# Routing rounds over ten packed slots instead of 24 tiles, in a fused attention and mixture-of-experts kernel

## Chip, cores and metric

The kernel runs on one core of one Trainium2 chip. The metric is the device time of one execution in microseconds, the median of several runs. All times of the kernel before are of that kernel on such a core.

## The reference

The program computes three layers, the second of which has a routing that depends on the data.

```python
# 1: attention with a decaying state, batch 4, 8 heads, 768 steps, head_dim 48
state = alpha[:, :, t, :, None] * state + outer(k[:, :, t], v[:, :, t])
y[:, :, t] = q[:, :, t] @ state
# 2: x = y as (3072 tokens, 384); E = 8 experts, F = 1024
logits = x @ w_gate                 # (3072, 8)
order = np.argsort(-logits.flatten())
for idx in order:                   # greedy, best pair first
    tok, e = idx // E, idx % E
    if assigned[tok] >= 0 or counts[e] >= cap: continue      # cap = 384
    assigned[tok] = e; counts[e] += 1
out[assigned == e] = relu(x[assigned == e] @ w1[e]) @ w2[e]
# 3: on every token, d_ff = 1536
g = x @ w_gate2
return (silu(g) * (x @ w_val)) @ w_out
```

So every expert ends up with exactly 384 tokens, and which ones depends on the order of 24,576 numbers.

## The kernel before

**Stages.** `attention` computes layer 1 and the logits, which stay on the chip as `logits`, 128 partitions by 24 tiles (`TILES`) by 8 experts; token 128·t + p lies on partition p in tile t. `layers` then takes the experts one after the other, in the order in which the routing fills them: layer 2 and layer 3 for the 384 tokens of that expert, and the rows go to `out`.

**Greedy routing as phases.** Since the best pairs go first, the routing is eight phases. In a phase every free token has one choice, its best expert among those with room (`choose`, L863 to L878: `best`, and `choice` as one of eight marked). The phase looks for the threshold on `best` at which the first expert becomes full, and assigns every token at or over it (`take`, L848). Phase 0, in front of the experts, uses four rounds of 31 cuts (`first_rounds_vector`). Phases 1 to 7 use three rounds (`FINE_ROUNDS`) of 99 cuts. A round has four parts: DVE compares `best` of each tile with all cuts (`compare`, L736, into `at_row`), PE counts per cut and expert with one small matmul for each of the 24 tiles (L891, into `ps_count`), DVE sees which cuts fill an expert (`find_full`, L744), PE sums these over partitions (L896), and DVE moves the base of the search (`raise_base`, L751). After `take`, the tokens of the newly full expert are ranked and listed: DVE writes a 128-wide row of marks per tile (L829, two halves of 12 tiles) and 24 matmuls (L911, two stretches of 12) turn them into token numbers, `slot_token`. On DVE nearly every small operation goes through `link`, which waits for the one before it.

**Where a phase runs.** The phase p+1 is spread over the work of expert p as steps s, in code written out by hand (`vector_step`, `tensor_step`, called by `route`). An expert has 20 places for a step. Places 0 to 7 come in the loop over m, the eight slices of layer 2: PE does `up(m+1)`, `down(m)` (9 matmuls each), then the step m; DVE makes `h_low(m)`, then the step m. Places 8 to 19 come in the loop over j, the twelve slices of layer 3: PE does `gate_and_value(j+1)` (18 matmuls), `project(j)` (9), then the step 8+j; DVE makes two products and `u_low(j)`, then the step. The phase takes 16 steps: compare, compare and count, find, three times; at s = `TAKE` = 9 `take`; then room and order (10), ranks (11), a first part of `at_row` (12) and a second (13), `slot_token` (14) and `choose` (15); the remaining small parts of phase p+1 lie in the same steps. `down(m)` waits for `h_low(m)` and `project(j)` for `u_low(j)`, so a step that keeps DVE too long makes PE wait.

**Other engines.** ACT makes the high parts of the numbers (each float32 matmul is three matmuls of split numbers), SP loads the weights. POOL subtracts to make `w_low` (L1438), starts the indirect transfers that gather the tokens of the next expert (L1430) and store those of the last (L1461), and in the first expert makes all of `gated_low` (L1296). `order[p]` tells SP which weights to load, at s = TAKE+1; `slot_token` releases the gather.

**A second way.** If at the end the routing did not come out exactly (`check_vector`: room left or below zero, a phase that filled no expert or two, a token left free), a second, exact routing and all the experts run again.

## Time and profile before

| | before |
|---|---|
| median of 3 runs | 874.03 us (872.48 to 876.46) |
| the profiled execution | 874.86 us |
| its span, first to last instruction | 873.0 us |
| PE busy | 835.8 us (96%) |
| DVE / ACT / POOL busy | 558.7 / 280.0 / 276.8 us |
| an expert, from the second on | 86.0 to 86.4 us |
| DMA, mean | 88 GB/s |

Attention fills the first 135 us or so, the first phase of the routing lies between it and about 168 us, and the eight experts fill the rest. To read it: the page's totals say which engine is busy, the stretches cut along the experts say whether that engine has any gap there, and the order of instructions in time says what a gap waits for. Spans of PE instructions overlap, so costs on PE are taken from the distance between starts.

### The profile page before, as it was taken

What the parts mean: (1) busy time and instruction counts of PE and PEld (TensorE: products, weight loads), DVE (VectorE), ACT (ScalarE), POOL (GpSimd) and SP (SyncE); (2) the same over time, 40 slices, a digit from 0 to 9 for tenths busy, and PEclk for the clock granted to TensorE, in tenths of its full rate; (3) what the DMA queues carried; (4) which work ended last, traced back from release to release, by engine and by line L of the source; (5) the groups of instructions that cost most, each with busy time, mean ns of one, the idle gap of its engine ahead of it and who ended that gap; (6) DMA issues with size and microseconds to landing.
All of it is one profiled execution on the core that took longest, in us unless ns stands there. A gap on an engine that the chain in (4) does not pass through costs nothing.

```text
span 873.0 us, 17172 instructions
## 1 busy us (share of the span) xinstructions
PE 835.8 (96%) x6425; PEld 792.0 (91%) x6425; DVE 558.7 (64%) x1065; ACT 280.0 (32%) x505; POOL 276.8 (32%) x263
## 2 busy tenths in 40 slices
PE   8899995699989999999999999999999999999995
PEld 5788884499989999999999999999999999999995
DVE  8999986757865665566556755675567556742332
ACT  1344443322323333333333333333333323333221
POOL 3222210179736041604150515051506050604001
PEclk9999997799999999999999999999999999999998
DMA  8899952500320041004100410031013001300000
GB/s 328 292 355 357 319 201 90 172 1 1 110 63 27 0 126 45 27 0 134 37 27 6 134 36 22 20 126 34 18 37 116 27 18 48 105 28 19 1 1 30
DMA packets 26001, 77.25 MB, mean 88 GB/s; under 512 B 3824, under 2 KB 10480, under 8 KB 23152
## 3 DMA queue, kind: packets, MB, share of 16 engines
q1 hardware_dynamic: 19440, 62.67, 20.8%
q0 software_dynamic: 3072, 9.44, 3.2%
q10 hardware_dynamic: 3456, 4.72, 1.5%
q8 instruction: 18, 0.29, 0.1%
q14 instruction: 15, 0.12, 0.0%
HBM read 67.38 MB, written 9.44 MB: 88 GB/s over the span
## 4 chain that ended last, share of the span: by engine, by line
PE 74%; DVE 6%; issue 2%; ACT 1%; DMA 0%; POOL 0%; POOLq 0%; DVEq 0%; ACTq 0%
PE ps_up L1634 44%; PE ps_acc L1634 27%; PE ps_turn_again L891 1%; DVE quick_at_row L829 1%; DVE u_low L1602 1%; DVE act_out L1599 1%; ACT u_high L1538 1%; PE ps_turn L1640 1%; PE ps_turn_again L911 0%; DVE act_out L1595 0%; PE ps_turn_again L771 0%; DVE quick_at_row L741 0%; DMA x_tok<-x_rows,slot_token 0%; PE ps_up L1640 0%; POOL x_tok L1493 0%
## 5 line engine op out<-in xcount | busy, mean ns | idle before, releaser
L1438 POOL TENSOR_TENSOR w_low<-w_raw,w_high 128x384 fp32r<-128x384 f32 x120 | 150.4, 1280 | 229.8 <-ACT w_high L1519 228.8
L1634 PE MATMUL ps_up<-z_high,gated_high 128*128 128x384 f32 x576 | 199.2, 346 | 0.2 <-DVE z_low L1590 0.2
L1634 PE MATMUL ps_up<-z_high,gated_low 128*128 128x384 f32 x576 | 195.5, 339 | 0.0
L1634 PE MATMUL ps_up<-z_low,gated_high 128*128 128x384 f32 x576 | 193.0, 335 | 0.0
L1538 ACT CAST u_high<-act_out 128x384 fp32r<-128x384 f32 x96 | 49.2, 513 | 190.9 <-DVE act_out L1599 190.9
L1634 PEld LDWEIGHTS ps_up<-z_high,gated_high 128*128 128x128 f32 x576 | 108.4, 188 | 0.6 <-issue 0.5
L1634 PEld LDWEIGHTS ps_up<-z_high,gated_low 128*128 128x128 f32 x576 | 108.5, 188 | 0.0
L1634 PEld LDWEIGHTS ps_up<-z_low,gated_high 128*128 128x128 f32 x576 | 108.3, 188 | 0.0
L1634 PE MATMUL ps_acc<-gated_high,u_high 128*128 128x384 f32 x288 | 97.6, 339 | 3.0 <-DVE u_low L1602 3.0
L1634 PE MATMUL ps_acc<-gated_high,u_low 128*128 128x384 f32 x288 | 97.1, 337 | 0.0
L1634 PE MATMUL ps_acc<-gated_low,u_high 128*128 128x384 f32 x288 | 97.0, 337 | 0.0
L1595 DVE TENSOR_TENSOR act_out<-ps_up,act_out 128x384 f32<-128x384 f32 x96 | 53.5, 557 | 67.5 <-ACT act_out L1535 63.8
L1461 POOL DMA_INDIRECT out<-o_tok,to_rows x24 | 26.0, 1085 | 220.6 <-ACT o_tok L1547 186.0
L1602 DVE TENSOR_TENSOR u_low<-act_out,u_high 128x384 fp32r<-128x384 f32 x96 | 58.3, 608 | 55.6 <-ACT u_high L1538 55.6
L1535 ACT ACTIVATE act_out<-ps_up 128x384 f32<-128x384 f32 x96 | 47.0, 490 | 129.9 <-PE ps_up L1634 129.9
L1584 DVE SCALAR_TENSOR_TENSOR h_low<-ps_up,h_high 128x384 fp32r<-128x384 f32 x64 | 35.6, 556 | 70.4 <-ACT h_high L1515 70.3
L1599 DVE TENSOR_TENSOR act_out<-act_out,ps_up 128x384 f32<-128x384 f32 x96 | 53.3, 555 | 38.6 <-PE ps_up L1634 37.2
L1634 PE MATMUL ps_up<-x_high,w_high 128*128 128x384 f32 x192 | 67.9, 354 | 1.1 <-ACT x_high L1511 1.1
L1519 ACT CAST w_high<-w_raw 128x768 fp32r<-128x768 f32 x64 | 53.3, 834 | 47.5 <-PE ps_acc L1634 35.0
L741 DVE SCALAR_TENSOR_TENSOR quick_at_row<-quick_best,quick_base,quick_fine_cuts 128x1485 bf16<-128x1485 f32 (+1 forms) x42 | 65.7, 1565 | 0.5
L1634 PE MATMUL ps_up<-x_high,w_low 128*128 128x384 f32 x192 | 65.2, 340 | 0.0
L1634 PE MATMUL ps_up<-x_low,w_high 128*128 128x384 f32 x192 | 65.1, 339 | 0.0
(179 smaller groups left out, 1467.6 us busy)
## 6 DMA issues: line engine op xcount, KB each, us to landing
w_raw<-in_experts SPq DMA_DIRECT2D x64, 384.0 KB, 3.0
qka_in<-in_qka SPq DMA_DIRECT2D x22, 1026.0 KB, 7.8
gated_raw<-in_gated SPq DMA_DIRECT2D x12, 576.0 KB, 6.8
v_in<-in_v SPq DMA_DIRECT2D x24, 192.0 KB, 7.0
x_rows<-y_rows ACTq DMA_DIRECT2D x24, 192.0 KB, 5.4
qka_in<-in_qka SPq DMA_DIRECT2D x2, 512.0 KB, 6.4
qka_in<-in_qka SPq DMA_DIRECT2D x1, 514.0 KB, 6.5
out<-o_tok,to_rows POOLq DMA_INDIRECT x24, 2.6
```

Of the source, the lines that this page charges most:

```text
L741: dve.scalar_tensor_tensor(out=self.at_row[:, tiles, 0:n], in0=self.best[:, tiles].unsqueeze(2).broadcast_to(tc), scalar=self.base[:, 0:1] ...
L829: dve.tensor_tensor(self.at_row[:, tiles, :], self.row[:, tiles].unsqueeze(2).broadcast_to(half), self.row_numbers[:, :].unsqueeze(1).broa ...
L1438: part = pool.tensor_tensor(w.low[:, m % RING, cols], w.raw[:, m % RING, cols], w.high[:, m % RING, cols].bitcast(F32), ALU.subtract)
L1461: pool.indirect_dma_start(out=out, out_offset=bass.IndirectOffsetOnAxis(ap=to_rows[:, t:t + 1], axis=0), in_=o_tok[:, t, :], in_offset=Non ...
L1519: act.copy(w.high[:, m % RING, :], w.raw[:, m % RING, :]).then_inc(w_high_ready, 1)
L1535: act.activation(act_out[:, j % 2, :], ps_up[j % 2][0][:, 0:CAP], ACT.Sigmoid).then_inc(sigm_ready, 1)
L1538: act.copy(u_high[:, j % 2, :], act_out[:, j % 2, :]).then_inc(u_high_ready, 1)
L1584: dve.scalar_tensor_tensor(out=h_low[:, m % 2, :], in0=ps_up[m % 2][0][:, 0:CAP], scalar=0.0, in1=h_high[:, m % 2, :].bitcast(F32), op0=AL ...
L1595: dve.tensor_tensor(act_out[:, j % 2, :], ps_up[j % 2][0][:, 0:CAP], act_out[:, j % 2, :], ALU.mult).then_inc(silu_ready, 1)
L1599: dve.tensor_tensor(act_out[:, j % 2, :], act_out[:, j % 2, :], ps_up[j % 2][1][:, 0:CAP], ALU.mult).then_inc(gated_ready, 1)
L1602: dve.tensor_tensor(u_low[:, j % 2, :], act_out[:, j % 2, :], u_high[:, j % 2, :].bitcast(F32), ALU.subtract).then_inc(u_low_ready, 1)
L1634: mm = pe.matmul(acc, lhs[a], rhs[b], start=(first and i == 0), stop=(last and i == 2))
```

## The change

From phase 1 on, the rounds no longer go over 24 tiles. Two new steps at the front of the phase (`SEARCH = 2`) pack the free tokens of each partition into ten slots. Step 0: `free` marks tokens whose `best` is a real number, a running sum gives each its place 1, 2, ..., `held` marks for slot j the tile whose free token has place j, and `number` is the choice as a number 1 to 8. Step 1: two products with `held` and two sums give `slot_best` and `slot_number`, and one comparison gives `slot_choice`. The compare then covers ten slots in one instruction and the count is ten matmuls. Compare and count lie in one step now, so a round has two steps instead of three. `TAKE` is 8 instead of 9, and each later step runs one place earlier. The matmuls of the listing, 12 in step TAKE+3 and 12 in TAKE+4 before, all run in TAKE+4. A partition with more than ten free tokens would have the rest left out of the counts.

```diff
-FINE_TILES = (slice(0, 15), slice(15, TILES))
+SLOTS = 10
...
-    TAKE = 3 * FINE_ROUNDS
+    SEARCH = 2
+    TAKE = SEARCH + 2 * FINE_ROUNDS
...
 # vector_step
-        n = s // 3
-        if s % 3 == 0 and 0 < s <= take:
+        n, finding = divmod(s - self.SEARCH, 2)
+        by_slot = [P, SLOTS, TILES]
+        if s == 0:
+
+            link(dve.tensor_scalar(self.free, self.best[:], -0.1 * BIG, None, ALU.is_gt))
+            link(dve.tensor_tensor_scan(self.place, self.free, self.zeros[:], 0.0, ALU.add, ALU.add))
+            link(dve.tensor_tensor(self.place, self.place, self.free, ALU.mult))
+            link(dve.tensor_tensor(self.held, self.place.unsqueeze(1).broadcast_to(by_slot),
+                                   self.numbers[:, 1:SLOTS + 1].unsqueeze(2).broadcast_to(by_slot), ALU.is_equal))
+            link(dve.tensor_tensor(self.numbered, self.choice[:],
+                                   self.numbers[:, 1:E + 1].unsqueeze(1).broadcast_to(te), ALU.mult))
+            link(dve.tensor_reduce(self.number, self.numbered, AX_X, ALU.add))
+        if s == 1:
+            for of, into in ((self.best[:, :], self.slot_best), (self.number, self.slot_number)):
+                link(dve.tensor_tensor(self.held_part, self.held, of.unsqueeze(1).broadcast_to(by_slot), ALU.mult))
+                link(dve.tensor_reduce(into[:], self.held_part, AX_X, ALU.add))
+            se = [P, SLOTS, E]
+            link(dve.tensor_tensor(self.slot_choice[:], self.slot_number[:, :].unsqueeze(2).broadcast_to(se),
+                                   self.numbers[:, 1:E + 1].unsqueeze(1).broadcast_to(se), ALU.is_equal))
+        if self.SEARCH < s <= take and not finding:
             self.raise_base(dve, self.rounds_before(p) + n, self.fine_cuts[:, n - 1, 0:1])
-        if s % 3 < 2 and s < take:
-            self.compare(dve, FINE_TILES[s % 3], self.fine_cuts[:, n, :])
-        if s % 3 == 2 and s < take:
+        if self.SEARCH <= s < take and not finding:
+            self.compare(dve, self.slot_best[:, :], slice(0, SLOTS), self.fine_cuts[:, n, :])
+        if self.SEARCH <= s < take and finding:
             self.find_full(dve, self.rounds_before(p) + n + 1, FINE_CUTS - 1)
...
 # tensor_step
-        if s % 3 == 1 and s < take:
-            for i, tiles in enumerate(FINE_TILES):
-                pe.wait_ge(self.over_cut_ready, 2 * self.rounds_before(p) + 2 * n + i + 1)
-                for t in range(tiles.start, tiles.stop):
-                    mm = pe.matmul(self.ps_count, self.at_row[:, t, :], self.choice[:, t, :],
-                                   start=(t == 0), stop=(t == TILES - 1))
+        if self.SEARCH <= s < take and not finding:
+
+            pe.wait_ge(self.over_cut_ready, ROUNDS + self.rounds_before(p) + n + 1)
+            for j in range(SLOTS):
+                mm = pe.matmul(self.ps_count, self.at_row[:, j, :], self.slot_choice[:, j, :],
+                               start=(j == 0), stop=(j == SLOTS - 1))
...
-        if s in (take + 3, take + 4):
-            i = s - take - 3
-            pe.wait_ge(self.at_row_ready, 2 * p + i + 1)
+        if s == take + 4:
+            for i in range(2):
+                pe.wait_ge(self.at_row_ready, 2 * p + i + 1)
```

Three places in the order of instructions show it; the numbers of lines shift by up to 30 in the kernel after. On PE, in the loop over m, the first count stands behind `down(1)` before:

```order
L1634 MATMUL ps_acc<-h_low,w_high 128x384
L889 ISA
L891 MATMUL ps_turn_again<-quick_choice,quick_at_row 128x8 x15
L889 REGISTER_ALU
L891 MATMUL ps_turn_again<-quick_choice,quick_at_row 128x8 x9
L1700 REGISTER_ALU
L1634 MATMUL ps_up<-x_high,w_high 128x384
```

and behind `down(2)` in the kernel after:

```order
L1664 MATMUL ps_acc<-h_low,w_high 128x384
L919 ISA
L921 MATMUL ps_turn_again<-quick_slot_choice,quick_at_row 128x8 x10
L1730 REGISTER_ALU
L1664 MATMUL ps_up<-x_high,w_high 128x384
```

Two waits and 24 matmuls became one wait and ten. On DVE, at the start of an expert, before:

```order
L1584 SCALAR_TENSOR_TENSOR h_low<-ps_up,h_high 128x384
L741 SCALAR_TENSOR_TENSOR quick_at_row<-quick_best,quick_base,quick_fine_cuts 128x15x99
L1583 REGISTER_ALU
L1584 SCALAR_TENSOR_TENSOR h_low<-ps_up,h_high 128x384
L741 SCALAR_TENSOR_TENSOR quick_at_row<-quick_best,quick_base,quick_fine_cuts 128x9x99
```

and after (the register and ISA rows are the waits of `link`; the scratch tiles lie in unused columns of `at_row` and bear its name):

```order
L1614 SCALAR_TENSOR_TENSOR h_low<-ps_up,h_high 128x384
L799 TENSOR_SCALAR quick_at_row<-quick_best 128x24
L694 ISA
L800 SCALAR_TENSOR_TENSOR quick_at_row<-quick_at_row,quick_zeros 128x24
L694 REGISTER_ALU
L801 TENSOR_TENSOR quick_at_row<-quick_at_row 128x24
L694 REGISTER_ALU
L802 TENSOR_TENSOR quick_at_row<-quick_at_row,quick_numbers 128x240
L694 REGISTER_ALU
L804 TENSOR_TENSOR quick_at_row<-quick_choice,quick_numbers 128x192
L694 REGISTER_ALU
L806 TENSOR_REDUCE quick_at_row<-quick_at_row 128x24
```

A compare of 15 tiles in the first place has become six small operations, and five more stand in the second. On DVE, behind the first `u_low` of layer 3 (j = 0), before:

```order
L1595 TENSOR_TENSOR act_out<-ps_up,act_out 128x384
L1599 TENSOR_TENSOR act_out<-act_out,ps_up 128x384
L1602 TENSOR_TENSOR u_low<-act_out,u_high 128x384
L747 REGISTER_ALU
L748 TENSOR_TENSOR quick_fills<-ps_turn_again,quick_room_or_big 99x8
```

and after:

```order
L1625 TENSOR_TENSOR act_out<-ps_up,act_out 128x384
L1629 TENSOR_TENSOR act_out<-act_out,ps_up 128x384
L1632 TENSOR_TENSOR u_low<-act_out,u_high 128x384
L765 SCALAR_TENSOR_TENSOR quick_base<-ps_turn_again,quick_fine_cuts,quick_base 128x1
L694 REGISTER_ALU
L882 TENSOR_SCALAR quick_is_over<-quick_best,quick_base 128x24
L694 REGISTER_ALU
L883 TENSOR_TENSOR quick_got<-quick_choice,quick_is_over 128x192
```

The find of the last round was there; now the last `raise_base` and `take` are, which stood behind `u_low` of j = 1 before.

## Rows read from the trace of the kernel before

**Rows 1.** page, busy time of the engines (share of the span).
```profile
PE 835.8 (96%) x6425; PEld 792.0 (91%) x6425; DVE 558.7 (64%) x1065; ACT 280.0 (32%) x505; POOL 276.8 (32%) x263
```

**Rows 2.** first, second expert: us; PE, PEld, DVE, ACT, POOL busy; clock; DMA.
```profile
172.00:262.39 90.39, 86.21 (x572) 83.23 (x571) 61.84 (x103) 26.88 (x49) 63.30 (x57) 1.00 0.15 48
262.39:348.80 86.41, 86.41 (x581) 84.76 (x580) 53.08 (x104) 28.46 (x50) 27.02 (x24) 1.00 0.16 50
```

**Rows 3.** timeline of PE, waits in the first expert (start, us, what [idle, releaser]).
```profile
217.47 0.19 PE L904 MATMUL ps_turn_again<-quick_mine,quick_below 128*128 128x24 bf16 x1 [1.24 <-DVE quick_mine L800]
...
221.37 0.41 PE L1634 MATMUL ps_acc<-gated_high,u_high 128*128 128x384 f32 x1 [0.42 <-DVE u_low L1602]
...
248.58 0.41 PE L1634 MATMUL ps_acc<-gated_high,u_high 128*128 128x384 f32 x1 [2.28 <-DVE u_low L1602]
```

**Rows 4.** timeline of PE, second expert, around its first count.
```profile
270.09 0.76 PE L891 MATMUL ps_turn_again<-quick_choice,quick_at_row 128*128 128x8 bf16 x24
...
270.97 0.34 PE L1634 MATMUL ps_up<-x_high,w_low 128*128 128x384 f32 x1
271.14 0.34 PE L1634 MATMUL ps_up<-x_low,w_high 128*128 128x384 f32 x1
```

**Rows 5.** timeline of PE, second expert, first half of its listing.
```profile
316.93 0.46 PE L911 MATMUL ps_turn_again<-quick_token_parts,quick_at_row 128*128 128x6 bf16 x12
...
317.50 0.34 PE L1634 MATMUL ps_up<-z_high,gated_low 128*128 128x384 f32 x1
```

**Rows 6.** timeline of DVE, start of the second expert.
```profile
264.54 0.56 DVE L1584 SCALAR_TENSOR_TENSOR h_low<-ps_up,h_high 128x384 fp32r<-128x384 f32 x1 [1.48 <-ACT h_high L1515]
265.01 1.76 DVE L741 SCALAR_TENSOR_TENSOR quick_at_row<-quick_best,quick_base,quick_fine_cuts 128x1485 bf16<-128x1485 f32 x1
...
267.15 1.14 DVE L741 SCALAR_TENSOR_TENSOR quick_at_row<-quick_best,quick_base,quick_fine_cuts 128x891 bf16<-128x891 f32 x1
```

**Rows 7.** DVE groups of the second expert (busy us, mean ns | idle).
```profile
L876 DVE TENSOR_TENSOR quick_fine_cuts<-quick_numbers,quick_fine_step 128x297 f32<-128x297 f32 x1 | 0.5, 471 | 0.0
...
L869 DVE TENSOR_REDUCE quick_best<-quick_limited 128x24 f32<-128x192 f32 x1 | 0.4, 353 | 0.0
...
L811 DVE TENSOR_TENSOR quick_rank<-quick_rank,quick_mine 128x24 f32<-128x24 f32 x1 | 0.2, 184 | 0.0
```

**Rows 8.** timeline of PE, second expert, beginnings: down(1), up(4), project(1).
```profile
268.52 0.33 PE L1634 MATMUL ps_acc<-h_high,w_high 128*128 128x384 f32 x1
...
273.99 0.42 PE L1634 MATMUL ps_up<-x_high,w_high 128*128 128x384 f32 x1
...
300.90 0.34 PE L1634 MATMUL ps_acc<-gated_high,u_high 128*128 128x384 f32 x1
```

**Rows 9.** timeline of POOL, second expert.
```profile
270.98 1.99 POOL L1438 TENSOR_TENSOR w_low<-w_raw,w_high 128x384 fp32r<-128x384 f32 x2
...
317.47 3.30 POOL L1438 TENSOR_TENSOR w_low<-w_raw,w_high 128x384 fp32r<-128x384 f32 x2 [1.43 <-ACT w_high L1519]
```

**Rows 10.** timeline of DVE, first expert, around take.
```profile
202.97 0.56 DVE L1602 TENSOR_TENSOR u_low<-act_out,u_high 128x384 fp32r<-128x384 f32 x1 [0.58 <-ACT u_high L1538]
...
203.94 0.56 DVE L1595 TENSOR_TENSOR act_out<-ps_up,act_out 128x384 f32<-128x384 f32 x1
...
206.13 0.64 DVE L1602 TENSOR_TENSOR u_low<-act_out,u_high 128x384 fp32r<-128x384 f32 x1 [0.58 <-ACT u_high L1538]
...
207.72 1.12 DVE L853 TENSOR_TENSOR quick_got<-quick_choice,quick_is_over 128x192 bf16<-128x192 bf16 x1
...
210.91 0.56 DVE L1595 TENSOR_TENSOR act_out<-ps_up,act_out 128x384 f32<-128x384 f32 x1
```

**Rows 11.** timeline of DVE, second expert, the same operations.
```profile
298.38 0.36 DVE L853 TENSOR_TENSOR quick_got<-quick_choice,quick_is_over 128x192 bf16<-128x192 bf16 x1
298.77 0.50 DVE L856 TENSOR_REDUCE quick_got_rows<-quick_got 128x8 bf16<-128x192 bf16 x1
...
299.58 0.26 DVE L861 TENSOR_TENSOR quick_assigned<-quick_assigned,quick_got 128x192 bf16<-128x192 bf16 x1
```

More of the change, by code:

```diff
@@ L510 @@
 STEPS = (1 << BITS) - 1
-QUICK_LINKS = 38
+QUICK_LINKS = 49
 EXACT_LINKS = 8 + 4 + 6 * (DIGITS - 1) + 17
@@ L584, in __init__ @@
         self.at_row = sb("at_row", [P, TILES, P], BF16)
+        self.slot_best = sb("slot_best", [P, SLOTS])
+        self.slot_number = sb("slot_number", [P, SLOTS])
+        self.slot_choice = sb("slot_choice", [P, SLOTS, E], BF16)
+        words = self.at_row[:, SLOTS:TILES, :].rearrange("p a b -> p (a b)").bitcast(F32)
+        self.held = words[:, 0:SLOTS * TILES].rearrange("p (j t) -> p j t", j=SLOTS)
+        self.held_part = words[:, SLOTS * TILES:2 * SLOTS * TILES].rearrange("p (j t) -> p j t", j=SLOTS)
+        rest = words[:, 2 * SLOTS * TILES:]
+        self.numbered = rest[:, 0:TILES * E].rearrange("p (t e) -> p t e", t=TILES)
+        self.free, self.place, self.number = (rest[:, TILES * (E + n):TILES * (E + n + 1)] for n in range(3))
         self.lows = sb("lows", [P, B, CH - 1])
@@ L735, in rounds_before, with compare @@
         return FINE_ROUNDS * p + ROUNDS - FINE_ROUNDS
-    def compare(self, dve, tiles, cuts):
+    def compare(self, dve, best, tiles, cuts):
         n = cuts.shape[-1]
         tc = [P, tiles.stop - tiles.start, n]
-        dve.scalar_tensor_tensor(out=self.at_row[:, tiles, 0:n], in0=self.best[:, tiles].unsqueeze(2).broadcast_to(tc),
+        dve.scalar_tensor_tensor(out=self.at_row[:, tiles, 0:n], in0=best.unsqueeze(2).broadcast_to(tc),
                                  scalar=self.base[:, 0:1], in1=cuts.unsqueeze(1).broadcast_to(tc),
@@ L761, in first_rounds_vector @@
             for i in range(2):
-                self.compare(dve, slice(i * TILES // 2, (i + 1) * TILES // 2), self.cuts[:, n, :])
+                tiles = slice(i * TILES // 2, (i + 1) * TILES // 2)
+                self.compare(dve, self.best[:, tiles], tiles, self.cuts[:, n, :])
             self.find_full(dve, n + 1, CUTS - 1)
@@ L832, in vector_step @@
         if s == take + 5:
[L833 removed]
+            dve.wait_ge(self.tokens_ready, p + 1)
             with self.nc.allow_low_precision(reason="token numbers up to N are exact"):
```

13 lines of the change are left out of this document (6 added, 7 removed).

## The prediction, made blind

> **What bounds the kernel now.** I read the page first: TensorE is busy for 96% of the span and VectorE for 64% [rows 1]. A share over the whole span mixes stages, so I cut it along the experts. From its first `up` to its last `project` the second expert takes 86.41 us, and PE is busy for all 86.41 of them, at a granted clock of 1.00, the upper of its two levels, 2.4 GHz [rows 2]. The five experts after it look the same. There is no gap on PE to close in there: a change pays by what it takes out of PE's stream, and costs what it adds in waits. The first expert is different: PE is busy 86.21 of 90.39 us [rows 2], and the timeline of PE says why. It waits 1.24 us for the `mine` of the routing, then 0.42 and 2.28 us for `u_low` [rows 3]. There VectorE is late, and it is the only expert in which POOL is busy for most of the time (63.30 us against 27.02 [rows 2]). So there are two questions: how many nanoseconds of PE one small matmul is worth, and whether VectorE's new work stays inside its cover.
>
> **What leaves PE.** A count of 24 matmuls starts at 270.09 and the second matmul behind it starts at 270.97. Ordinary starts lie 0.17 apart (270.97 to 271.14), so the count costs 0.88 - 0.17 = 0.71 us [rows 4]. Half a listing, 12 matmuls of the same kind, costs 317.50 - 316.93 - 0.17 = 0.40 us [rows 5]. The difference, 0.31 us for 12, is 0.026 us for each matmul, and 0.09 us is left as the price of switching over and back. Ten matmuls should then cost 0.35 us, and a count gives back 0.36 us. There are 3 rounds in each of 7 phases: 21 x 0.36 = **7.6 us**. The listing as one stretch costs 0.71 in place of 0.80 us: 7 x 0.09 = **0.6 us**. The second matmul of each round (L896) only moves. Phase 0 keeps its rounds; its listing waits for the same two halves as before, so nothing changes there. Together 8.2 us, all on the path, as PE has no other gap.
>
> **What VectorE gets, from the second expert on.** The packing has eleven operations. None has a row of its own, so I bound them by the nearest: 0.18 us for 24 elements, 0.35 us for a sum over 192, 0.47 us for 297 [rows 7]; 240 elements lie between, about 0.41. With 0.03 us between linked operations (298.38 + 0.36 to 298.77 [rows 11]) step 0 takes 3 x 0.2 + 0.41 + 2 x 0.36 + 0.2 = 1.9 us, between 1.7 and 2.2, and step 1 takes 4 x 0.41 + 0.25 + 0.15 = 2.0 us. `h_low(0)` ends at 265.10 [rows 6], so step 0 ends at 267.0, `h_low(1)` at 267.6, and `down(1)` starts at 268.52 [rows 8]: cover 0.9 us. Step 1 then ends at 269.6 and `h_low(2)` at 270.2, while `down(2)` comes two times nine matmuls after `down(1)`, at 271.6: cover 1.4 us. The compare of ten slots has 990 elements, between 1.14 us for 891 and 1.76 us for 1485, nearest the lower: 1.25 us [rows 6], and it replaces both. Priced at nothing.
>
> In layer 3 each step stands one place earlier, so `take` comes behind `u_low(0)` instead of `u_low(1)`. In the second expert `take` and the `raise_base` ahead of it run from 297.9 to 299.84 [rows 11], 2.0 us. In the new place the next product waits 1.6 us for it, `u_low(1)` ends at about 299.5, and `project(1)` starts at 300.90 [rows 8]: cover 1.4 us, nothing on PE. `order` and `slot_token` are ready one step earlier. That makes nobody faster, because SP's loads and POOL's gather are paced by free weight buffers and by POOL's own `w_low`.
>
> **What it does to the first expert.** There `take` lasts from 206.77 (206.13 + 0.64) to 210.91, 4.1 us [rows 10]. In its old place the product after it would have been due one slice of PE later than the one at 203.94, that is 27 x 0.175 = 4.7 us, at about 208.7; it came 2.2 us late. In the new place `take` starts when `u_low(0)` ends, 203.53, the product is due at 203.94 [rows 10], and it comes some 3.7 us late. VectorE thus reaches the heavy steps of room and ranks 1.5 us further behind, while PE reaches them 1.1 us earlier (three counts). I carried that chain on with the times of the rows: waits of 0.3, 1.3, 1.9 and 0.6 us in place of 1.24 and 0.42, some 2.4 us more. Against this, the last routing step now stands one place earlier, and the wait of 2.28 us behind it [rows 3] shrinks or goes. The ends are 2.4 us lost and 2.3 us won; I take half of the late wait as gone: **1.2 us lost**.
>
> **Sum.** 8.2 - 1.2 = 7.0 us. Against the profiled execution, 874.86 us (span 873.0), that is 867.9; that execution is 0.8 us over the median of the runs, 874.03, so the median should be 867.0.
>
> **Contention, a rule against the row.** First the rows: the same product of 192 elements takes 0.36 us in the second expert [rows 11] and 1.12 us in the first [rows 10], where POOL subtracts without a pause, while nothing else about it differs. The Trainium skill, "SBUF — State Buffer", section "Who interferes with whom", states that a VectorE instruction with two inputs in SBUF and a GpSimd instruction that reads SBUF exclude each other for a whole instruction, and that `tensor_reduce` is free of it. By that rule most operations of the packing can be held, and the trace agrees with the rule in the 0.76 us between the two rows. Whether it bites depends on what POOL does during steps 0 and 1. The first `w_low` of the second expert starts at 270.98 [rows 9], after both steps (269.6). In the first expert POOL is subtracting by step 1, at most one instruction of 1.0 us in the way, within the cover of 1.4 us.
>
> **Rivals.**
> 1. *The packing and the compare push POOL or VectorE out of cover in the later experts.* `w_low` for `up(4)` is done at 270.98 + 1.99 = 272.97, and `up(4)` starts at 273.99 [rows 8, 9]; after the change it starts 0.36 us earlier, at 273.6. The compare of step 2 now lies at 270.2 to 271.5, so `w_low` may begin only at 271.5 and end at 273.5: 0.1 us of cover. If VectorE gets between its two halves, they take 3.30 us, as the pair at 317.47 did [rows 9], and end at 274.3. PE then waits 0.7 us in six experts, 4.2 us: 867.0 + 4.2 = 871.2. For it speaks the thin cover, against it that the compare is likely under way before POOL begins. Chance 0.20.
> 2. *The first expert wins.* If VectorE catches up before its last routing step, PE keeps its savings and the 2.28 us [rows 3] go as well: 874.0 - 8.2 - 2.3 = 863.5. The cheaper compare (1.25 for 2.90 us in each round) speaks for it, the chain above against it. Chance 0.18.
> 3. *Slower: the packing is held in every expert.* If the stores that POOL starts in steps 0 and 1 hold VectorE as its subtraction does, four or five operations of step 0 each take 0.76 us more, up to 3.8 us, of which 0.9 us is covered. PE waits 2.9 us in each of seven experts, 20 us: about 887. It decides from 1.8 us of waits per expert on, where the 8.2 us and the 4.4 us of a visible loss are used up. Against it: what POOL has in those steps are starts of stores, and its first subtraction comes at 270.98 [rows 9]. Chance 0.05.
> 4. *It doesn't do what it says.* If a partition had over ten free tokens, a phase would take too many, the check at the end would find it, and all the experts would run again: over 1500 us. I followed the reference's own assignment on its inputs of seed 0: 248 tokens are free after phase 0, at most 5 of them in one partition. Chance 0.01.
>
> **How the numbers follow.** The case of the sum has a chance of 0.56 and its own range from 865 to 869. The range from 863.0 to 871.5 takes in rivals 1 and 2, and leaves out rivals 3 and 4 and their edges. A measurement of this kernel can tell about 0.5% from no change, 4.4 us, so "faster" ends at 869.7. Faster: 0.53 of the first case, all of rival 2, a quarter of rival 1: 0.76. Slower: rivals 3 and 4: 0.06. Within 0.5%: 0.18.
>
> **What would show it.** The group of counts should have 210 matmuls for 504, and a count should cost about 0.35 us between starts. An expert should last 85.3 us for 86.4, with PE busy throughout. The first expert should show larger waits of PE for `mine` and for `u_low` around 205 to 220 us, and a smaller one before 250. The packing's groups should sum to 3.9 us per expert. A wait of `down(1)` for `h_low` or of `up(4)` for `w_low` in every expert would make the prediction wrong, and so would a price per matmul that falls well under 0.026 us at ten in a row.

## The result, and the profile after

The kernel after takes **907.13 us** (median of 3 runs, 906.96 to 907.15), against 874.03 before: a ratio of **1.0375** (95% interval 1.0344 to 1.0406). It is slower, and far outside the predicted range of 863.0 to 871.5 us.

The page of the kernel after: span, busy time, two of the rows of 40 slices, and the chain that ended last.

```profile
span 905.3 us, 16689 instructions
...
PE 840.9 (93%) x6131; PEld 795.5 (88%) x6131; DVE 577.3 (64%) x1121; ACT 280.3 (31%) x505; POOL 251.8 (28%) x263
...
PE   8899993897998999899989998999899989999996
...
PEclk9999996899998999899989998999899989999998
...
PE ps_up L1664 41%; PE ps_acc L1664 23%; DVE quick_at_row L752 5%; DMA out<-o_tok,to_rows 1%; PE ps_turn_again L921 1%; DVE quick_at_row L809 1%; PE ps_turn_again L941 1%; DVE z_low L1620 1%; PE ps_turn L1670 0%; ACT z_high L1562 0%; DVE quick_at_row L859 0%; PE ps_turn_again L783 0%; ACT h_high L1545 0%; DMA x_tok<-x_rows,slot_token 0%; DVE act_out L1629 0%
```

PE executes 294 instructions fewer than before [rows 1], as announced, and yet its busy share fell from 96% to 93%. From the thirteenth slice on (about 272 us, the second expert), one slice in every four has a lower PE digit and a lower clock digit. Four slices are about one expert, so something happens once per expert. A compare, L752, now holds 5% of the chain. The waits of PE in the kernel after (us in total, times, the longest) name the place:

```profile
PE ps_turn_again L921 <- DVE quick_at_row L752: 25.7, 6, 4.3
...
PE ps_acc L1664 <- DVE u_low L1632: 3.5, 4, 1.5
PE ps_turn_again L934 <- DVE quick_mine L830: 3.3, 2, 1.8
```

The first line has no counterpart before. In each of the experts two to seven the first count, the one of step 2, waits 4.28 us for its compare. Here is DVE in the second expert (start, us, what):

```profile
268.82 0.24 DVE L812 TENSOR_TENSOR quick_slot_choice<-quick_slot_number,quick_numbers 128x80 bf16<-128x80 f32 x1
269.19 0.56 DVE L1614 SCALAR_TENSOR_TENSOR h_low<-ps_up,h_high 128x384 fp32r<-128x384 f32 x1
269.66 7.53 DVE L752 SCALAR_TENSOR_TENSOR quick_at_row<-quick_slot_best,quick_base,quick_fine_cuts 128x990 bf16<-128x990 f32 x1
277.12 0.55 DVE L1614 SCALAR_TENSOR_TENSOR h_low<-ps_up,h_high 128x384 fp32r<-128x384 f32 x1
...
283.18 1.25 DVE L752 SCALAR_TENSOR_TENSOR quick_at_row<-quick_slot_best,quick_base,quick_fine_cuts 128x990 bf16<-128x990 f32 x1
```

The same instruction takes 1.25 us in the next round and 7.53 us here. Below, a VectorE operation is called *held* where it takes longer than its usual time while POOL works. POOL at that time:

```profile
269.37 0.96 POOL L1491 DMA_INDIRECT out<-o_tok,to_rows  x1 [2.43 <-DMA out<-o_tok,to_rows]
270.35 5.79 POOL L1468 TENSOR_TENSOR w_low<-w_raw,w_high 128x384 fp32r<-128x384 f32 x6
283.81 1.50 POOL L1468 TENSOR_TENSOR w_low<-w_raw,w_high 128x384 fp32r<-128x384 f32 x1 [7.67 <-ACT w_high L1549]
```

The compare starts while POOL starts its last store. POOL then subtracts six times without a gap, up to 276.14, and the compare ends 1.05 us after that, at 277.19. PE at that time (at 277.25, the count; behind it, big matmuls):

```profile
272.63 0.34 PE L1664 MATMUL ps_acc<-h_low,w_high 128*128 128x384 f32 x1
277.25 0.43 PE L921 MATMUL ps_turn_again<-quick_slot_choice,quick_at_row 128*128 128x8 bf16 x10 [4.28 <-DVE quick_at_row L752]
...
278.00 0.52 PE L1664 MATMUL ps_up<-x_high,w_low 128*128 128x384 f32 x1
278.32 0.52 PE L1664 MATMUL ps_up<-x_low,w_high 128*128 128x384 f32 x1
```

The windows of the same stretch (from, to, length; PE, PEld, DVE, ACT, POOL busy; granted clock, share of DMA, GB/s):

```profile
273.00:277.20 4.20, 0.00 (x0) 0.00 (x0) 4.20 (x2) 0.83 (x1) 3.14 (x4) 0.73 0.00 0
277.20:280.00 2.80, 2.75 (x18) 2.75 (x19) 0.79 (x3) 0.00 (x0) 0.00 (x0) 0.50 0.00 0
280.00:282.00 2.00, 2.00 (x9) 2.00 (x7) 0.56 (x1) 0.49 (x1) 0.00 (x0) 0.56 0.00 0
282.00:284.00 2.00, 2.00 (x13) 1.84 (x13) 1.04 (x2) 0.84 (x1) 0.19 (x1) 1.00 0.00 0
```

The wait has a second price. PE is idle for 4.28 us, its granted clock falls to 0.50, the lower level (1.2 GHz), and matmuls start 0.32 us apart instead of 0.17 until shortly before 282. From there on the clock is back at 1.00, 2.4 GHz. The later experts repeat this: from the first `up` of one expert to the first `up` of the next, the experts two to seven take 91.49 to 92.17 us, against 86.39 to 86.41 before. Summed over the six, that is 33.2 us. The first expert got 0.22 us shorter (93.32 to 93.10). So the six account for the whole loss (32.3 us between the spans).

**Why POOL's run has no gap now.** POOL in the second expert of the kernel before, around the second compare:

```profile
270.98 3.92 POOL L1438 TENSOR_TENSOR w_low<-w_raw,w_high 128x384 fp32r<-128x384 f32 x4
275.06 4.09 POOL L1438 TENSOR_TENSOR w_low<-w_raw,w_high 128x384 fp32r<-128x384 f32 x2 [0.17 <-ACT w_high L1519]
```

DVE of the same kernel there:

```profile
274.44 2.04 DVE L741 SCALAR_TENSOR_TENSOR quick_at_row<-quick_best,quick_base,quick_fine_cuts 128x1485 bf16<-128x1485 f32 x1
```

POOL has to wait for ACT's third `w_high` behind four subtractions, 0.17 us, and the compare of 15 tiles that arrived at 274.44 is done at 276.48. ACT makes the `w_high` that goes with `w_low` for a weight buffer after PE has left that buffer, behind a `down`. In the kernel after, `down(2)` stands ahead of the first count, so ACT has the third `w_high` ready in time (each is enough for two subtractions) and POOL has six subtractions to do instead of four. The fourth `w_high` needs `down(3)`, which stands behind the count, which needs the compare, which needs POOL to pause: a ring that opens only when POOL has run out of ready work.

### The profile page after: what moved, and what is told of

Same layout as the page of the kernel before. It is cut to its first block, busy times and chain, and to the rows that moved or that the text cites. A ratio compares the mean times of both kernels' runs of the same rounds, so it can differ in the third digit from the quotient of the medians.

```text
span 905.3 us, 16689 instructions
## 1 busy us (share of the span) xinstructions
PE 840.9 (93%) x6131; PEld 795.5 (88%) x6131; DVE 577.3 (64%) x1121; ACT 280.3 (31%) x505; POOL 251.8 (28%) x263
## 4 chain that ended last, share of the span: by engine, by line
PE 66%; DVE 12%; issue 3%; ACT 1%; DMA 1%; POOL 1%; POOLq 0%; DVEq 0%; ACTq 0%
PE ps_up L1664 41%; PE ps_acc L1664 23%; DVE quick_at_row L752 5%; DMA out<-o_tok,to_rows 1%; PE ps_turn_again L921 1%; DVE quick_at_row L809 1%; PE ps_turn_again L941 1%; DVE z_low L1620 1%; PE ps_turn L1670 0%; ACT z_high L1562 0%; DVE quick_at_row L859 0%; PE ps_turn_again L783 0%; ACT h_high L1545 0%; DMA x_tok<-x_rows,slot_token 0%; DVE act_out L1629 0%
## 5 line engine op out<-in xcount | busy, mean ns | idle before, releaser
L1468 POOL TENSOR_TENSOR w_low<-w_raw,w_high 128x384 fp32r<-128x384 f32 x120 | 130.5, 1114 | 290.5 <-ACT w_high L1549 290.2
L1664 PE MATMUL ps_up<-z_high,gated_high 128*128 128x384 f32 x576 | 195.9, 340 | 1.4 <-DVE z_low L1620 1.4
L1664 PE MATMUL ps_up<-z_high,gated_low 128*128 128x384 f32 x576 | 192.6, 334 | 0.0
L1491 POOL DMA_INDIRECT out<-o_tok,to_rows x24 | 23.9, 997 | 216.4 <-ACT o_tok L1577 180.4
L1664 PE MATMUL ps_up<-x_high,w_high 128*128 128x384 f32 x192 | 71.3, 372 | 1.5 <-ACT x_high L1541 1.1
L1545 ACT ACTIVATE h_high<-ps_up 128x384 fp32r<-128x384 f32 x64 | 31.5, 492 | 122.0 <-PE ps_up L1664 122.0
L1664 PE MATMUL ps_up<-x_low,w_high 128*128 128x384 f32 x192 | 68.5, 357 | 0.0
L1664 PE MATMUL ps_up<-x_high,w_low 128*128 128x384 f32 x192 | 68.3, 356 | 0.0
```

Source lines behind the costliest of these rows:

```text
L1468: part = pool.tensor_tensor(w.low[:, m % RING, cols], w.raw[:, m % RING, cols], w.high[:, m % RING, cols].bitcast(F32), ALU.subtract)
L1491: pool.indirect_dma_start(out=out, out_offset=bass.IndirectOffsetOnAxis(ap=to_rows[:, t:t + 1], axis=0), in_=o_tok[:, t, :], in_offset=Non ...
L1545: act.activation(h_high[:, m % 2, :], ps_up[m % 2][0][:, 0:CAP], ACT.Relu).then_inc(h_high_ready, 1)
L1664: mm = pe.matmul(acc, lhs[a], rhs[b], start=(first and i == 0), stop=(last and i == 2))
```

## The experiments

Two explanations stood against each other. One: the compare, which has two large inputs in SBUF, is held beside POOL's subtractions up to the end of POOL's unbroken run, so that the end of the run decides. The other: each compare loses a fixed amount or a fixed number of POOL instructions, or the packing makes VectorE late by itself. A separate question was how much of the loss is the wait and how much the clock.

**1. The compare one step later.**

```diff
-    SEARCH = 2
+    SEARCH = 3
```

> The kernel after with one empty routing step between the packing and the first compare (SEARCH = 3, TAKE = 9), so that compare starts some 3 us later in an expert, in the middle of POOL's run of w_low and not beside its last store start. Theory A (the compare is caught because it starts beside the store start that POOL follows at once with subtractions): the compare takes 1.25 us plus at most one subtraction, 1.0 us, PE keeps its clock, the 8.2 us of the counts show: about 866 us. Theory B (any compare that meets POOL's unbroken run of w_low is held to the end of the run): it is held from 272.8 to 276 or 278, PE waits 1 to 3 us per expert and its clock may fall: 873 to 890 us. Theory C (the ten slots or the packing themselves are slow): like after, about 907 us.

Measured: 876.55 us, ratio 1.003 (1.0019 to 1.0041). DVE in the second expert:

```profile
271.39 4.85 DVE L752 SCALAR_TENSOR_TENSOR quick_at_row<-quick_slot_best,quick_base,quick_fine_cuts 128x990 bf16<-128x990 f32 x1
```

POOL of the same kernel there:

```profile
269.34 5.85 POOL L1468 TENSOR_TENSOR w_low<-w_raw,w_high 128x384 fp32r<-128x384 f32 x6
```

The compare arrives 2 us into the run and ends, as in the kernel after, 1.05 us behind it (275.19 and 276.24). So the time of the end goes with the end of the run, not with the start of the compare. The count is due one step later, so PE waits only 1.20 to 1.26 us, and its clock does not fall behind that wait; the experts two to seven take 86.66 to 86.73 us.

**2. The compare's big input from PSUM.**

```diff
+        self.ps_best = bank[:, 480:480 + SLOTS]
...
-            for of, into in ((self.best[:, :], self.slot_best), (self.number, self.slot_number)):
+            for of, into in ((self.best[:, :], self.ps_best), (self.number, self.slot_number)):
...
-            self.compare(dve, self.slot_best[:, :], slice(0, SLOTS), self.fine_cuts[:, n, :])
+            self.compare(dve, self.ps_best, slice(0, SLOTS), self.fine_cuts[:, n, :])
```

> The kernel after with slot_best in PSUM, so that the compare has one large input in SBUF and one in PSUM; same steps, same order, same start. Theory of the shared port (only an instruction with two SBUF inputs is excluded by POOL): the compare is not held, 1.25 us, PE has no wait in experts two to seven, about 867 us as the prediction had it. Rival (the hold is of the VectorE instruction as such, whatever its inputs, or of its output): the compare still takes 7.5 us and the time stays at 907 us.

Measured: 870.26 us, ratio 0.9962 (0.9949 to 0.9975). POOL's run is as long as in the kernel after. The new tile lies in the PSUM bank of the other small results and bears its name, `ps_turn_again`. DVE in the second expert:

```profile
272.07 1.24 DVE L753 SCALAR_TENSOR_TENSOR quick_at_row<-ps_turn_again,quick_base,quick_fine_cuts 128x990 bf16<-128x990 f32 x1
```

POOL of the same kernel there:

```profile
272.76 5.86 POOL L1469 TENSOR_TENSOR w_low<-w_raw,w_high 128x384 fp32r<-128x384 f32 x6
```

With one of its two large inputs in PSUM the compare is not held, though POOL begins the same six subtractions while it runs, and the experts take 85.14 to 85.16 us. Nothing else about it changed, so for this compare the second SBUF input is the condition. But the first expert took 95.44 us instead of 93.10, and there a `u_low`, with two SBUF inputs, was held. DVE in the first expert:

```profile
200.28 9.79 DVE L1633 TENSOR_TENSOR u_low<-act_out,u_high 128x384 fp32r<-128x384 f32 x1 [0.58 <-ACT u_high L1569]
```

POOL of the same kernel there:

```profile
194.22 15.43 POOL L1327 TENSOR_TENSOR gated_low<-gated_raw,gated_high 128x384 fp32r<-128x384 f32 x16
```

PE of the same kernel there:

```profile
210.21 0.66 PE L1665 MATMUL ps_acc<-gated_high,u_high 128*128 128x384 f32 x1 [7.98 <-DVE u_low L1633]
```

POOL's run ends at 209.65, the `u_low` at 210.07.

**3. PE kept busy during the wait**, to price the clock alone.

```diff
+            if s == self.SEARCH:
+                for _ in range(20):
+                    pe.matmul(self.warm_out, self.warm_w, self.warm_x, start=True, stop=True)
             pe.wait_ge(self.over_cut_ready, ROUNDS + self.rounds_before(p) + n + 1)
...
```

> The kernel after with 20 matmuls of 512 columns that compute nothing needed (4.3 us) on PE ahead of the wait for the first compare. It separates the wait itself from the clock. Theory: the hold of the compare stays (7.5 us) and PE loses the same 4.3 us per expert, but its clock stays at 1.00 behind it, which gives back the 2.3 to 3 us per expert of half clock; the first expert, which had no such wait, loses 4.3 us: 907 - 6 x 2.7 + 4.3 = about 895 us. If the clock plays no part: about 911 us.

Measured: 895.76 us, ratio 1.0246 (1.0231 to 1.0261). The compare takes 7.55 us, nearly the 7.53 of the kernel after, and the count comes 4.66 us behind the start of the last `down` matmul (4.62 there). DVE in the second expert:

```profile
274.08 7.55 DVE L752 SCALAR_TENSOR_TENSOR quick_at_row<-quick_slot_best,quick_base,quick_fine_cuts 128x990 bf16<-128x990 f32 x1
```

The granted clock stays at 1.00 behind it, and the experts two to seven take 89.55 to 89.65 us for 91.49 to 92.17. So the clock behind the wait is worth 1.9 us in the second expert, 2.3 in the third and 2.4 to 2.5 in the others; the rest of the loss is the wait. The first expert, which had no such wait, takes 97.39 us for 93.10: there the 20 matmuls cost their full 4.3 us, as expected.

**4. Three sums ahead of the compare** (their results are not used).

```diff
...
+        if s == self.SEARCH:
+            for _ in range(3):
+                link(dve.tensor_reduce(self.number, self.logits[:], AX_X, ALU.max))
```

> The kernel after with three sums over 192 logits (0.39 us each, one SBUF input, result unused) on VectorE ahead of the first compare of each phase, so that it starts 1.2 us later, at about 270.8 in the second expert's time, inside POOL's first subtraction behind the store start. Theory A1 (caught only beside the store start): the compare waits for one subtraction at most, about 867 us. Theory A2 (caught as well during the first subtraction, as the u_low of the first expert before at 244.57 suggests) or theory B (whole run): it lasts until 276.1 again, about 6.3 us long, and the time stays near 907 us.

Measured: 907.22 us in one run. DVE in the second expert:

```profile
269.62 1.12 DVE L818 TENSOR_REDUCE quick_at_row<-logits 128x24 f32<-128x192 f32 x3
270.77 6.38 DVE L752 SCALAR_TENSOR_TENSOR quick_at_row<-quick_slot_best,quick_base,quick_fine_cuts 128x990 bf16<-128x990 f32 x1
```

PE of the same kernel there:

```profile
277.21 0.41 PE L924 MATMUL ps_turn_again<-quick_slot_choice,quick_at_row 128*128 128x8 bf16 x10 [4.28 <-DVE quick_at_row L752]
```

Starting 1.1 us later costs nothing: compare and wait end where they did. The sums have one input. They take 0.37 us each with their gaps, the first two beside the start of the store and the third inside POOL's first subtraction, which begins at 270.32. The time that the packing takes is not what is paid for.

**5. Both remedies, 1 and 2, together.** The edits are those two.

> Both of the last: one empty step ahead of the first compare (so that take and all later steps keep the places they had before) and slot_best in PSUM. The compare has no part in the shared port, and the first expert has the steps of layer 3 where the kernel before had them. If the counts are worth what experts two to seven of e2 show (85.15 us for 86.41), those give 6 x 1.26 = 7.6 us, and the first expert, which was at 92.2 us in e1 and 95.4 us in e2 (93.3 before), about 1 us: 874.0 - 8.6 = about 865.5 us. If an u_low of the first expert is held through POOL's run as in e2 (9.8 us there), up to 8 us of it are lost again: 873 us.

Measured: 872.57 us, ratio 0.9985 (0.9975 to 0.9996). The experts take 85.30 to 85.39 us, the first one 98.48: again a `u_low`, held 9.55 us, with PE waiting 7.74 us for it. What the experts two to seven give back, the first loses again to a hold in another place.

**6. A gap for POOL: ACT makes one high part later.**

```diff
-                        act.wait_ge(w_used, RING * e + m + 1)
+                        act.wait_ge(w_used, RING * e + (m + 2 if m == 2 else m + 1))
```

> The kernel after; ACT makes the high part for w_low(6) only after down(3), which comes after the first count. Theory (the held compare is let in when POOL runs out of ready subtractions; before, the high part of slice 6 came too late for an unbroken run, and the kernel after brought it forward): POOL has four subtractions ready, the compare is let in at the end of the fourth, 1.9 us sooner, and lasts 5.6 us, PE waits 2.3 to 2.4 in place of 4.28 us: 907 - 6 x 1.9 = about 895 us, a little less still if the clock falls for less long. Rival (the hold has a length of its own, whatever POOL has ready): 7.5 us and 907 us or more.

Measured: 894.42 us, ratio 1.0254 (1.0228 to 1.0281). POOL in the second expert:

```profile
271.34 3.89 POOL L1468 TENSOR_TENSOR w_low<-w_raw,w_high 128x384 fp32r<-128x384 f32 x4
```

DVE of the same kernel there:

```profile
270.63 5.65 DVE L752 SCALAR_TENSOR_TENSOR quick_at_row<-quick_slot_best,quick_base,quick_fine_cuts 128x990 bf16<-128x990 f32 x1
```

PE of the same kernel there:

```profile
276.34 0.41 PE L921 MATMUL ps_turn_again<-quick_slot_choice,quick_at_row 128*128 128x8 bf16 x10 [2.39 <-DVE quick_at_row L752]
```

Two subtractions fewer in the run, and the compare is 1.9 us shorter, the wait too. The length of the run sets the price, as the ring says.

The clock is less regular. The experts two and three take 90.15 and 90.24 us, the experts four to seven 88.56 to 88.64, with the same wait of 2.39 us in each. The 4 us behind that wait in the experts two to five (from, to, length; PE, PEld, DVE, ACT, POOL busy; granted clock, share of DMA, GB/s):

```profile
276.34:280.34 4.00, 4.00 (x25) 4.00 (x26) 0.74 (x3) 0.00 (x0) 0.00 (x0) 0.71 0.00 0
366.49:370.49 4.00, 4.00 (x23) 4.00 (x24) 0.74 (x3) 0.00 (x0) 0.00 (x0) 0.57 0.00 0
456.71:460.71 4.00, 4.00 (x32) 3.84 (x33) 0.74 (x3) 0.32 (x1) 0.00 (x0) 1.00 0.00 0
545.29:549.29 4.00, 4.00 (x32) 3.84 (x33) 0.74 (x3) 0.32 (x1) 0.00 (x0) 1.00 0.00 0
```

So the same wait cost some 1.6 us of clock in two experts and none in four. Why is not shown.

**7. POOL waits for the compare.** The subtractions of the weights' second half, behind the last store, begin only when the first compare of the phase is done (experts one to seven).

```diff
             def split_rest(e):
+                if not again and not (isinstance(e, int) and e == E - 1):
+                    pool.wait_ge(quick.over_cut_ready, 2 * ROUNDS + FINE_ROUNDS * e + 1)
```

> The kernel after; from the first expert to the seventh POOL starts its four w_low of the second half only when the first compare of the phase is done. The compare still starts beside the same store start, with the same two SBUF inputs, and only the subtractions behind it wait. Theory (it is the run of subtractions that holds it): 1.25 us for the compare, no wait for the count, w_low(4) at most 0.1 us late for up(4): about 868 us. Rival (the store start itself holds it): the compare stays far above 1.25 us and the count still waits.

Measured: **866.24 us** (865.65 to 867.29), ratio **0.991** (0.9896 to 0.9925), the fastest of all and faster than both kernels. DVE in the second expert:

```profile
269.74 1.24 DVE L752 SCALAR_TENSOR_TENSOR quick_at_row<-quick_slot_best,quick_base,quick_fine_cuts 128x990 bf16<-128x990 f32 x1
```

POOL of the same kernel there:

```profile
269.43 0.96 POOL L1493 DMA_INDIRECT out<-o_tok,to_rows  x1 [2.43 <-DMA out<-o_tok,to_rows]
271.16 5.86 POOL L1468 TENSOR_TENSOR w_low<-w_raw,w_high 128x384 fp32r<-128x384 f32 x6 [0.77 <-DVE quick_at_row L752]
```

PE of the same kernel there:

```profile
272.87 0.41 PE L921 MATMUL ps_turn_again<-quick_slot_choice,quick_at_row 128*128 128x8 bf16 x10
273.20 0.44 PE L1666 MATMUL ps_up<-x_high,w_high 128*128 128x384 f32 x1
```

The compare starts beside the same start of a store as in the kernel after and takes 1.24 us: the store's start does not hold it, the subtractions do. POOL stands still for 0.77 us, and that removes the hold, the wait and the lost clock. The experts two to seven take 85.18 to 85.22 us. The first takes 93.04, nearly as in the kernel after (93.10), though POOL's subtractions begin 3 us later there too, at 179.34 instead of 176.32.

One thing stays without an explanation. In the kernel after, the compare had 0.69 us to itself ahead of the first subtraction, and yet it ended 1.05 us behind the run, just as in experiment 1, where it arrived in the middle of the run. The head start was worth nothing.

**8. A small operation in the kernel before**, a maximum of two tiles in SBUF. Its result is overwritten before it is used.

```diff
...
+            if s == 2:
+                link(dve.tensor_tensor(self.before[:], self.best[:], self.zeros[:], ALU.max))
```

> The kernel BEFORE, with one maximum of two SBUF tiles of 24 elements (0.18 us by itself, result unused) on VectorE at the end of step 2, which starts at about 271.3 in the second expert's time, inside POOL's first subtraction behind the stores. No slots and no packing. Theory (any VectorE instruction with two SBUF inputs that comes in there is held until POOL's run breaks, at 274.9 before): it lasts about 3.6 us, h_low(3) is late by 1.8 us and PE hardly waits, 874 to 876 us. Rival (it is the compare, its size or its form, that loses): it lasts at most 1.2 us, 874 us.

Measured: 874.64 us in one run. DVE in the second expert:

```profile
270.54 3.24 DVE L791 TENSOR_TENSOR quick_before<-quick_best,quick_zeros 128x24 f32<-128x24 f32 x1
```

POOL of the same kernel there:

```profile
269.82 3.91 POOL L1440 TENSOR_TENSOR w_low<-w_raw,w_high 128x384 fp32r<-128x384 f32 x4
273.90 6.23 POOL L1440 TENSOR_TENSOR w_low<-w_raw,w_high 128x384 fp32r<-128x384 f32 x4 [0.16 <-ACT w_high L1521]
```

An operation of 24 elements takes 3.24 us: it ends at 273.78, in the 0.16 us in which POOL waits for ACT. No slots and no packing are needed for the hold. It cost only 0.2 to 0.3 us per expert (86.60 to 86.68 us), as nothing on PE was waiting for it.

**9. Six slots**, on the kernel of experiment 7 (`SLOTS = 6`). **10. The listing in one stretch**, alone in the kernel before (the diff of the listing shown ahead, nothing else).

> The kernel of e7 (POOL's second half behind the first compare) with six slots for ten; on these inputs no partition has more than five free tokens after phase 0. It measures the price of a small matmul with nothing held: 4 matmuls fewer in each of 3 rounds of an expert. At 0.026 us each, an expert takes 0.31 us less (84.9 for 85.2 us) and the run 7 x 0.31 = 2.2 us less than e7: 864.1 us. If short stretches cost more for the switch than for their matmuls, the time stays near 866 us.

> The kernel BEFORE with the listing change alone: all 24 matmuls of it in the later of its two steps, rounds and take untouched. By the prediction's second term an expert takes 0.09 us less (86.32 for 86.41 us), and the run about 0.6 us less. Rival: PE now waits for the second half of at_row, or slot_token comes late; then an expert takes longer.

Measured: 875.65 us (ratio 1.0014, 1.0001 to 1.0026) with six slots, 874.8 us in one run with the listing alone. The listing made an expert some 0.05 us shorter (86.34 to 86.37 for 86.39 to 86.41), about half of the 0.09 expected; in the whole time, 874.8 us for a median of 874.13 of the kernel before, it can't be seen. The six slots missed: the experts took 85.35 to 85.37 us, not less than with ten. The three counts themselves were cheaper, as expected. With six matmuls PE loses 0.26 us per count, with ten 0.35, with 24 0.71. What came back was elsewhere, in the pace of the big matmuls. PE in the second expert of the kernel before, from the first matmul of a `project` to the first of the second one after it:

```profile
325.61 0.34 PE L1634 MATMUL ps_acc<-gated_high,u_high 128*128 128x384 f32 x1
...
335.06 0.34 PE L1634 MATMUL ps_acc<-gated_high,u_high 128*128 128x384 f32 x1
```

The same piece in experiment 7:

```profile
324.28 0.33 PE L1666 MATMUL ps_acc<-gated_high,u_high 128*128 128x384 f32 x1
...
333.64 0.33 PE L1666 MATMUL ps_acc<-gated_high,u_high 128*128 128x384 f32 x1
```

Both pieces hold the same 54 matmuls and nothing else, and PE has no gap in either: 9.45 / 54 = 175 ns between starts before, 9.36 / 54 = 173.3 ns in experiment 7, at a granted clock of 1.00. Experiments 8, 9 and 10 have the slower pace, with starts mostly 170 to 182 ns apart. The kernel after and experiments 1 to 7 have the even one, 1 and 5 not in every stretch. Averaged over all 449 or so ordinary starts of an expert, the two paces are 174.55 and 173.55 ns (before, experiment 7). In experiment 9 the first expert, at 99.42 us, was also worse: a `u_low` was held 4.61 us, and PE waited 3.36 us for it.

**11. and 12. Is it where the tiles lie?** Unused tiles move all later ones: in the kernel before, by as much as the change's slot tiles do, and in the kernel with six slots, to where they lie with ten.

```diff
+        self.unused = sb("unused", [P, 60])     # 11
...
+        self.unused = sb("unused", [P, 24])     # 12
```

> The kernel before with one unused tile of 60 words per partition (240 bytes) behind at_row, where the change has its three slot tiles (240 bytes too). Nothing is computed differently; every tile allocated later lies where it lies in the kernel after. Why: inside the experts the big matmuls start 175.2 ns apart on average and unevenly (170 to 179) in the traces of before, e8, e10 and e9, and 173.3 ns apart and evenly in those of after and of e1 to e7. So of the 1.2 us that an expert of e7 is shorter than one of before, the small matmuls may explain only about 0.8. Theory P (where the tiles lie sets the pace): here the starts are 173.3 ns apart, an expert lasts 86.0 us for 86.41, and the kernel takes about 871 us (0.4 us in each of eight experts). Theory Q (the pace comes with the instruction stream, or with the slots): 175.2 ns, 86.4 us and 874 to 875 us.

> e9 (six slots, POOL behind the compare) with one unused tile of 24 words per partition (96 bytes) behind the slot tiles, so that these and it take 240 bytes as in the kernel after. Theory P (where the tiles lie sets the pace): 173.3 ns between the big matmuls for e9's 175.2, experts of 84.9 us for 85.36, as the three counts are 0.1 us cheaper each than with ten slots; the total is e9's 875.7 less 3 to 4 us, 872, if its first expert stays at 99.4 us, and 866 or less if that expert comes back to 93. Theory Q: 85.36 us and 875 us.

Measured: 874.04 us, ratio 0.9997 (0.9988 to 1.0007), and 874.26 us, ratio 0.9999 (0.9988 to 1.001). The pace of these pieces stayed at 175.1 ns in both. In experiment 11 the experts took 86.37 to 86.41 us; in 12 they took 85.20, 0.16 less than in 9, though not the 84.9 of theory P (the average over all ordinary starts went from 174.8 to 174.4 ns). The first expert of 12 took 97.82 us, with a `u_low` held 4.60 us as in 9. Theory P fails on the pace. Theory Q, that the pace comes with the stream of instructions, is what is left, and no run tested it.

## Why the prediction was wrong, point by point

**The step that failed** is the overlap of the first compare with POOL's subtractions. In the sum the compare stood at 1.25 us, "priced at nothing", and the only price for meeting POOL was that of rival 1. The prediction placed the compare at 270.2 and let `w_low` wait for it ("the compare is likely under way before POOL begins"), with 0.7 us for PE if it came out otherwise. The compare came at 269.66 and was indeed under way 0.7 us ahead of the first subtraction, and it was held nonetheless, up to the end of six subtractions: 7.53 us. So the chance of 0.20 went with a price of 0.7 us per expert where the runs show 4.28 us of wait and 1.9 to 2.5 us of clock. (Even in its own terms that price was low: a `w_low` that begins at 271.5 and takes 3.30 us ends at 274.8, not at 274.3, which gives 1.2 us.) Rival 3, "slower", had its place wrong, too: the small operations of the packing met nothing, the compare behind them did. And the two waits that were named as signs of being wrong, of `down(1)` for `h_low` and of `up(4)` for `w_low`, did not come in the experts two to seven; the wait that came is that of the count for its compare, which was not on the list.

**The rule of the hold.** The prediction took from the Trainium skill, "SBUF — State Buffer", section "Who interferes with whom", that a VectorE instruction with two SBUF inputs and a GpSimd instruction that reads SBUF exclude each other for one whole instruction, and priced it so: one subtraction in the way, 0.76 us. Experiments 2 and 4 agree with the rule on who is held: not a compare with one input in PSUM, not a sum. How long a hold lasts is another matter, and there the runs disagree with the prediction's price. Operations were held through runs of four, six and ten or so subtractions in a row: 3.24 us in experiment 8, 7.53 in the kernel after, 9.79 in experiment 2.

**It could have been read in the trace of before.** The prediction put the wait of 2.28 us [rows 3] down to VectorE being late. Two rows of the first expert show why it was late. DVE:

```profile
244.57 3.87 DVE L1602 TENSOR_TENSOR u_low<-act_out,u_high 128x384 fp32r<-128x384 f32 x1 [0.58 <-ACT u_high L1538]
```

POOL of the same kernel there:

```profile
244.13 3.87 POOL L1438 TENSOR_TENSOR w_low<-w_raw,w_high 128x384 fp32r<-128x384 f32 x4
```

An operation of 0.56 us took 3.87 us, until 0.44 us behind the end of POOL's four subtractions. The rows on which the prediction leaned instead [rows 10], 1.12 us for 0.36, show a milder form, in which VectorE gets in between two of POOL's instructions. Both forms stand in the same trace, and one was taken for the only one.

**The order of instructions.** The prediction saw that `down(2)` now precedes the first count, and used it only for PE's cover. It did not ask what else `down(2)` releases: the weight buffer, by it ACT's cast, and by that two more subtractions in POOL's run. Experiment 6 takes those two out again and gets 1.9 us of the hold back.

**What leaves PE: right in its terms, less so in its sum.** A count of ten costs 0.35 us, as worked out. Between the kernel before and experiment 7, where no first compare is held, one of the experts two to seven is about 1.2 us shorter, against a forecast of 3 x 0.36 + 0.09 = 1.17. That agreement is partly luck. Summed over the places where PE does small matmuls, an expert gives back 0.75 us (4.20 to 3.44 us): the counts 0.98, as the first one costs 0.42, and the listing 0.10, less 0.30 for the find that now stands where the layers change. PE there waits 0.2 us for `z_low`, which the count of 24 had covered before. The other 0.45 us came from the pace of the big matmuls, 449 starts at 1.0 ns less each, which the prediction did not have.

**VectorE's packing: right.** Its eleven operations took 0.17 to 0.41 us each, with their gaps 1.84 and 1.99 us in the second expert, where 1.9 and 2.0 were foreseen. The waits of PE in the experts two to seven show no `down` waiting for `h_low`.

**The first expert: right in size, by two misses that cancel.** The waits of PE for the routing and for `u_low` are 5.3 us in the kernel after for 4.2 before, 1.1 us more, for a forecast of 1.2. But the early waits grew by some 3 us (1.28, 1.49, 0.42 and 1.52 us for 1.24 and 0.42) where 2.4 were foreseen, and the late one shrank from 2.28 to 0.39 us, 1.9 us won where 1.2 were taken. The three cheaper counts and the listing paid for the rest, and the expert came out 0.22 us shorter.

**The sum**, without the hold, was 867.0 us; experiment 7, the change plus one wait on POOL, takes 866.24. By the part on what leaves PE, that closeness is in part luck too.

## What to carry to other kernels

Before moving a VectorE operation with two SBUF inputs, look for what GpSimd does at its new time, and price it by the whole unbroken run of GpSimd behind it, not by one instruction. Look in the old trace for VectorE operations far over their usual time, and at what ends with them. If the operation is one on which GpSimd's own next input depends, the two form a ring. Here a semaphore wait on GpSimd of under a microsecond opened it, and one input in PSUM avoided it, though both kernels with that input in PSUM (experiments 2 and 5) met a long hold of `u_low` in the first expert. A wait on PE of 4.28 us cost up to 2.5 us more in clock.

## What the runs showed of the hardware

- A hold of VectorE lasts as long as GpSimd's instructions follow each other without a gap, in the cases shown: 7.53, 6.38, 5.65 and 4.85 us for 1.25, 9.79 for 0.56, 3.24 in experiment 8. A gap of 0.16 us was enough to end it there.
- In other places of the same traces VectorE got in at the next boundary of GpSimd's instructions [rows 10]. What decides between the two was not found. In the kernel after, the compare had even started 0.69 us ahead of the subtractions; beside the start of the store alone it takes 1.24 us (experiment 7).
- PE's pace at full granted clock has two values in the stretches compared, 173.3 ns and even, 175.1 to 175.3 ns and uneven (one stretch in each of experiments 1 and 5 lies between, at 174.2 to 175.0 ns); apart from those two, the same stretch shows the same one in each expert looked at of a kernel. It is worth 0.45 us per expert here and did not follow the place of the tiles (experiments 11 and 12). Its cause stays open.
- Six matmuls of 8 columns between big ones cost 0.26 us, ten 0.35, 24 0.71: 0.02 to 0.03 us each, and by an estimate from these some 0.1 us for each stretch of them.
- Behind a pause of PE of 4.28 us the granted clock was 0.50 to 0.56 for over 4 us, worth 1.9 to 2.5 us (kernel after against experiment 3). Behind a pause of 2.39 us it was 0.57 to 0.71 over 4 us in two experts and 1.00 in the others (experiment 6), and behind 1.20 to 1.26 us it did not fall (experiment 1).
